# One queue for the first loads, two score tiles ahead of the block means: a fused attention, mixture-of-experts and feed-forward kernel

## The reference, cut to what matters

```python
# q, k, v: [2, 8, 768, 64]; block 32, window 16
k_sum = k.reshape(B, H, nb, 32, D).max(axis=3)       # 24 block maxima of the keys
v_sum = v.reshape(B, H, nb, 32, D).mean(axis=3)      # 24 block means of the values
scores_l = where(|i - j| < 16, scale * q @ k.T, -1e9)
scores_s = scale * q @ k_sum.T + log(32)
a = softmax(concat([scores_l, scores_s]))            # +1e-9 in the denominator
x = a @ concat([v, v_sum])                           # -> [1536, 512]
logits = x @ w_gate; noisy = logits + log1p(exp(x @ w_noise)) * noise
top 2 of 8 experts per token, softmax of the two noisy logits
x = sum over the two: weight * (relu(x @ w1[e]) @ w2[e])     # 512 -> 1024 -> 512
out = (s * relu(x @ w_in)**2 + b) @ w_out                    # 512 -> 2048 -> 512
```

## Time and profile before

| | us |
|---|---|
| median of 3 runs | 733.51 |
| the profiled execution, whole | 733.46 |
| its span in the trace | 731.8 |
| PE busy in the span | 692.8 (95%) |
| DVE, ACT, POOL busy | 263.7, 215.0, 294.2 |
| mean granted TensorE clock | 0.978 of full |

### The profile page before, as it was taken

How to read it: one execution, slowest core, us unless ns; L and a number is a source line. 1 busy time by engine, 2 the same in 40 slices (tenths; PEclk the granted TensorE clock), 3 DMA queues, 4 the chain that set the end, 5 groups by cost and what they waited for, 6 DMA issues and landing times.

```text
span 731.8 us, 10317 instructions
## 1 busy us (share of the span) xinstructions
PE 692.8 (95%) x4019; PEld 566.6 (77%) x4022; DVE 263.7 (36%) x535; ACT 215.0 (29%) x503; POOL 294.2 (40%) x273
## 2 busy tenths in 40 slices
PE   8888867999999999999999998999999999999993
PEld 3466653878888888887989897888888888888883
DVE  3557777581111211211111235845505235152220
ACT  0678961112031221212121212412315123242120
POOL 0001554478978667394979750502031020200002
PEclk9999977999999999999999999999999999999997
DMA  9994986963969679393989695942011020100001
GB/s 234 238 249 118 305 299 222 366 239 118 330 209 356 210 255 357 117 394 129 331 273 365 196 384 224 374 154 58 0 61 56 0 58 1 57 1 1 0 1 57
DMA packets 57291, 135.35 MB, mean 185 GB/s; under 512 B 9437, under 2 KB 11741, under 8 KB 57245
## 3 DMA queue, kind: packets, MB, share of 16 engines
q0 software_dynamic: 30288, 88.13, 35.4%
q1 hardware_dynamic: 25760, 44.24, 19.7%
q10 hardware_dynamic: 1197, 2.36, 1.3%
HBM read 108.99 MB, written 24.67 MB: 183 GB/s over the span
## 4 chain that ended last, share of the span: by engine, by line
PE 79%; DMA 7%; DVE 4%; SPq 4%; ACT 2%; issue 2%; POOL 1%; POOLq 0%; DVEq 0%
PE ps L335 24%; PE ps L336 24%; PE ps L337 24%; DMA v_all<-in_v_dram 3%; DMA yg<-y_sorted,ord_i 2%; PE ps L1313 2%; SPq L316 1%; PE ps L1261 1%; PE ps L1244 1%; POOL x_sorted L480 1%; SPq L350 1%; SPq L311 1%; ACT prob L597 1%; DMA y_sorted<-ysb 1%; PE ps L1399 1%
## 5 line engine op out<-in xcount | busy, mean ns | idle before, releaser
L460 POOL TENSOR_TENSOR w_lo<-w_raw,w_hi 128x1024 fp32r<-128x1024 f32 x56 | 133.5, 2425 | 27.8 <-DVE w_lo L812 15.1
L1038 DVE SCALAR_TENSOR_TENSOR h_lo<-ps,h_hi 128x448 fp32r<-128x448 f32 (+1 forms) x64 | 38.1, 598 | 206.6 <-ACT h_hi L647 206.6
L335 PE MATMUL ps<-w_hi,h_hi 128*128 128x512 f32 x232 | 93.2, 402 | 0.0
L335 PE MATMUL ps<-x_hi,w_hi 128*128 128x448 f32 (+1 forms) x256 | 91.6, 358 | 1.3 <-DVE x_lo L1032 1.3
L647 ACT ACTIVATE h_hi<-ps 128x448 fp32r<-128x448 f32 (+1 forms) x64 | 33.6, 525 | 196.3 <-PE ps L337 196.3
L336 PE MATMUL ps<-x_lo,w_hi 128*128 128x448 f32 (+1 forms) x256 | 91.1, 356 | 0.0
L337 PE MATMUL ps<-x_hi,w_lo 128*128 128x448 f32 (+1 forms) x256 | 91.0, 356 | 0.0
L336 PE MATMUL ps<-w_lo,h_hi 128*128 128x512 f32 x232 | 90.8, 392 | 0.0
L337 PE MATMUL ps<-w_hi,h_lo 128*128 128x512 f32 x232 | 90.8, 391 | 0.0
L1117 DVE SCALAR_TENSOR_TENSOR sqr<-relu,sbb 128x512 f32<-128x512 f32 x48 | 36.2, 754 | 113.0 <-ACT relu L700 112.2
L336 PE MATMUL ps<-y_lo,w_hi 128*128 128x512 f32 (+1 forms) x200 | 76.1, 381 | 0.0
(11 more groups left out here) (197 smaller groups left out, 1088.5 us busy)
## 6 DMA issues: line engine op xcount, KB each, us to landing
w_hi<-in_w_pieces_dram POOLq DMA_DIRECT2D x64, 512.0 KB, 14.1
w_raw<-in_w_pieces_dram POOLq DMA_DIRECT2D x56, 512.0 KB, 13.5
x_sorted<-zrow SPq DMA_DIRECT2D x8, 896.0 KB, 15.3
xb<-x_sorted SPq DMA_DIRECT2D x24, 256.0 KB, 8.0
y_sorted<-ysb SPq DMA_DIRECT2D x24, 256.0 KB, 2.0
w_raw<-in_w_pieces_dram SPq DMA_DIRECT2D x8, 512.0 KB, 5.8
w_hi<-in_w_in_dram POOLq DMA_DIRECT2D x8, 512.0 KB, 10.1
w_raw<-in_w_in_dram SPq DMA_DIRECT2D x8, 512.0 KB, 15.7
```

Of the source, the lines that this page charges most:

```text
L335: pe.matmul(acc, l_hi, r_hi, start=start, stop=False, skip_group_check=True)
L460: pool.tensor_tensor(piece(w_lo, slot, k), piece(w_raw, slot, k), piece(w_hi, slot, k).bitcast(F32), ALU.subtract).then_inc(pieces_split, 1)
L1038: dve.scalar_tensor_tensor(out=h_lo[:, at, i % FT, 0:rows], in0=ps[:, i % FT, 0:rows], scalar=0.0, in1=h_hi[:, at, i % FT, 0:rows].bitcast ...
```

## The change

SP now issues all first loads; ACT issues none. The values of batch 0 stand behind `ident`, first as 80 rows of each window (what the means need) and then the remaining 16 as a DMA of its own (`halo_in`). The values of batch 1 come ahead of its keys, and `noi` and `sbb` behind the first halves of its queries, with a semaphore `n_in` of their own that DVE waits for in `route_top`. On PE, `scores(0)`, `scores(1)` and `turn_probs(0)` come ahead of `means(0)`; the warm-up is 34, 8 and 6 matmuls in three places where it was 66 in one; the means of batch 0 go to PSUM banks 6 and 7, and sum over 80 rows. DVE, not ACT, copies the means of batch 0. The key maxima of batch 1 move from tiles 1, 2, 3, 4 to 2, 3, 3, 4. ACT's first act is a small copy, after the zeros of `zrow` are there.

```diff
--- before.py
+++ after.py
...
+MEAN_ROWS = HALF + 16
+MEAN_BANKS = ((6, 7), (2, 1))
+KEY_SUMS_AT = (2, 3, 3, 4)
...
+        n_in, halo_in = sem("n_in"), sem("halo_in")
...
@@ -298,10 +302,13 @@
         def overflow_steps(eng):
             return eng.value_load(t_last[0:1, 0:1], min_val=0, max_val=OVER)
 
-        def load_values(eng, b):
-            windows = bass.AP(tensor=v.tensor, offset=v[b].offset, ap=[[DM, HALF + 32], [HALF * DM, HPB - 1], [1, DM]])
+        def load_windows(eng, b, at, to, landed):
+            windows = bass.AP(tensor=v.tensor, offset=v[b, at].offset, ap=[[DM, to - at], [HALF * DM, HPB - 1], [1, DM]])
+            eng.dma_start(v_all[b][at:to, 0:HPB - 1, :], windows).then_inc(landed, 16)
+
+        def load_values(eng, b, rows):
             last = (HPB - 1) * HALF
-            eng.dma_start(v_all[b][0:HALF + 32, 0:HPB - 1, :], windows).then_inc(v_in[b], 16)
+            load_windows(eng, b, 0, rows, v_in[b])
             eng.dma_start(v_all[b][0:HALF, HPB - 1, :], v[b, last:last + HALF, :]).then_inc(v_in[b], 16)
             eng.wait_ge(init_ready, 1)
             eng.dma_start(v_all[b][HALF:WKEYS, HPB - 1, :], v[b, S:S + 2 * PAD, :]).then_inc(v_in[b], 16)
@@ -344,13 +351,15 @@
             sp.dma_start(msk[0:80, :], masks[0:80, :]).then_inc(m_in, 16)
             load_queries(sp, 0, 0)
             sp.dma_start(ident[:, :], consts[:, 0:P]).then_inc(id_in, 16)
+            load_values(sp, 0, MEAN_ROWS)
+            load_windows(sp, 0, MEAN_ROWS, HALF + 32, halo_in)
             load_queries(sp, 0, 1)
             sp.dma_start(wg[:, :, :], w_gate.rearrange("(k p) e -> p k e", p=P)).then_inc(g_in, 16)
-            sp.dma_start(noi[:, :, :], noise.rearrange("(t p) e -> p t e", p=P)).then_inc(g_in, 16)
-            sp.dma_start(sbb[:, :], s_b).then_inc(g_in, 16)
+            load_values(sp, 1, HALF + 32)
             load_keys(sp, 1)
-            load_values(sp, 1)
             load_queries(sp, 1, 0)
+            sp.dma_start(noi[:, :, :], noise.rearrange("(t p) e -> p t e", p=P)).then_inc(n_in, 16)
+            sp.dma_start(sbb[:, :], s_b).then_inc(n_in, 16)
             load_queries(sp, 1, 1)
             sp.wait_ge(init_ready, 2)
             clear_rows(sp, 0)
@@ -585,9 +594,8 @@
 
             def copy_means(b):
                 act.wait_ge(means_done, b + 1)
-                if b == 1:
-                    act.wait_ge(rows_done, 1)
-                act.activation(vs_sb[:, :], ps[:, 2, :], ACT.Copy).then_inc(vs_ready, 1)
+                act.wait_ge(rows_done, b)
+                act.activation(vs_sb[:, :], ps[:, MEAN_BANKS[b][0], :], ACT.Copy).then_inc(vs_ready, 1)
 
             def exps(s):
                 act.wait_ge(nb_ready, s + 1)
@@ -607,10 +615,10 @@
                 act.wait_ge(ln_in, g + 1)
                 act.activation(rt[:, R_LN, 0:to - at, :], rt[:, R_Y, 0:to - at, :], ACT.Ln).then_inc(ln_ready, 1)
 
-            load_values(act, 0)
+            act.wait_ge(init_ready, 2)
+            act.activation(gate[:, :], zrow[:, 0:NT], ACT.Copy)
             key_windows(0)
             key_windows(1)
-            copy_means(0)
             exps(0)
             ends = {to: g for g, (at, to) in enumerate(GROUP_OF)}
             for s in range(NT + 1):
@@ -802,9 +810,13 @@
                 dve.tensor_copy(sel[:, 0:NSUM].rearrange("p (c m) -> p c m", m=NSUM // KD),
                                 ident[:, :].rearrange("p (c m) -> p c m", c=KD)[:, :, 0:NSUM // KD]).then_inc(sel_ready, 1)
 
+            def copy_means(b):
+                dve.wait_ge(means_done, b + 1)
+                dve.tensor_copy(vs_sb[:, :], ps[:, MEAN_BANKS[b][0], :]).then_inc(vs_ready, 1)
+
             def mean_rows(b):
                 dve.wait_ge(rows_done, b + 1)
-                dve.tensor_copy(v_all[b][SUMS:COLS, 0:2 - b, :], bc(ps[SUMS:COLS, 3 - 2 * b, :], 2 - b, 1)).then_inc(rows_ready, 1)
+                dve.tensor_copy(v_all[b][SUMS:COLS, 0:2 - b, :], bc(ps[SUMS:COLS, MEAN_BANKS[b][1], :], 2 - b, 1)).then_inc(rows_ready, 1)
 
             def split_first(k):
                 dve.wait_ge(raw_first[k], 16)
@@ -859,6 +871,7 @@
                 n = to - at
                 dve.wait_ge(lg_ready, to)
                 dve.wait_ge(ln_ready, g + 1)
+                dve.wait_ge(n_in, 32)
                 link(dve.tensor_tensor(rt[:, R_SP, 0:n, :], rt[:, R_LN, 0:n, :], rt[:, R_C, 0:n, :], ALU.subtract))
                 link(dve.tensor_tensor(rt[:, R_N, 0:n, :], rt[:, R_SP, 0:n, :], noi[:, at:to, :], ALU.mult))
                 link(dve.tensor_tensor(rt[:, R_L, 0:n, :], rt[:, R_N, 0:n, :], lg[:, at:to, 0:E], ALU.add))
@@ -900,9 +913,8 @@
             key_sums(1)
             masks_to_bf16()
             select_rows()
+            maxima(0)
             token_numbers()
-            maxima(0)
-            mean_rows(0)
             for s in range(NT):
                 if s in (7, 10):
                     route_chosen(s // 10)
@@ -910,8 +922,12 @@
                     maxima(s + 1)
                 dve.wait_ge(turned, 2 * s + 1)
                 dve.tensor_copy(probT[0:COLS, 0:4, :], ps[0:COLS, 4, :].rearrange("p (h n) -> p h n", n=P)).then_inc(probT_even, 1)
-                if 1 <= s <= PAIRS:
-                    summary(1, s - 1)
+                if s == 0:
+                    copy_means(0)
+                    mean_rows(0)
+                for p in range(PAIRS):
+                    if s == KEY_SUMS_AT[p]:
+                        summary(1, p)
                 if s in (TPB - 2, TPB - 1):
                     key_sums(s + 2)
                 if s == 4:
@@ -1177,8 +1193,6 @@
                 pe.wait_ge(sums_ready, 2 * b + min(tt, 1) + 1)
                 if s >= 2:
                     pe.wait_ge(exps_done, 8 * (s - 1))
-                if s == 1:
-                    pe.wait_ge(rows_ready, 1)
                 if s == TPB - 1:
                     pe.wait_ge(vs_ready, 2)
                 if s == TPB:
@@ -1202,7 +1216,8 @@
                 pe.wait_ge(v_in[b], 48)
                 for r in range(HPT):
                     for c in range(KD):
-                        mm = pe.matmul(ps[c * 32:c * 32 + 32, 2, :], amean[0:WKEYS, r, :], v_all[b][0:WKEYS, c * HPT + r, :],
+                        mm = pe.matmul(ps[c * 32:c * 32 + 32, MEAN_BANKS[b][0], :], amean[0:MEAN_ROWS, r, :],
+                                       v_all[b][0:MEAN_ROWS, c * HPT + r, :],
                                        start=(r == 0), stop=(r == HPT - 1), skip_group_check=True)
                 mm.then_inc(means_done, 1)
 
@@ -1210,7 +1225,7 @@
                 if b == 0:
                     pe.wait_ge(sel_ready, 1)
                 pe.wait_ge(vs_ready, b + 1)
-                pe.matmul(ps[SUMS:P, 3 - 2 * b, :], sel[:, :], vs_sb[:, :], start=True, stop=True).then_inc(rows_done, 1)
+                pe.matmul(ps[SUMS:P, MEAN_BANKS[b][1], :], sel[:, :], vs_sb[:, :], start=True, stop=True).then_inc(rows_done, 1)
             def warm_up(count, bank):
 
                 pe.wait_ge(init_ready, 1)
@@ -1230,6 +1245,8 @@
                 b, tt = divmod(s, TPB)
                 if tt == 0:
                     pe.wait_ge(rows_ready, b + 1)
+                if s == 0:
+                    pe.wait_ge(halo_in, 16)
                 if tt == 1 - b:
                     pe.wait_ge(means_in[b][0], 16)
                 if tt == 3:
@@ -1255,7 +1272,7 @@
 
             def logits(t):
                 if t == 0:
-                    pe.wait_ge(g_in, 48)
+                    pe.wait_ge(g_in, 16)
                 pe.wait_ge(xT_ready, t + 1)
                 for k in range(KD):
                     mm = pe.matmul(ps[:, 7, 0:2 * E], xT[:, t % 2, k, :], wg[:, k, :], start=(k == 0), stop=(k == KD - 1))
@@ -1273,17 +1290,21 @@
                     mm = pe.matmul(acc, ones[:, :], before[:, t, :], start=False, stop=True)
                 mm.then_inc(rank_done, 1)
 
-            warm_up(66, 7)
+            warm_up(34, 7)
+            scores(0)
+            scores(1)
+            warm_up(8, 7)
+            turn_probs(0)
+            warm_up(6, 7)
             means(0)
-            scores(0)
             gather_means(0)
-            for s in range(NT):
+            values(0)
+            for s in range(1, NT):
                 if s + 1 < NT:
                     scores(s + 1)
-                if s >= 1:
-                    if s in (8, 11):
-                        pe.wait_ge(rank_read, 1 + s // 11)
-                    turn_x(s - 1)
+                if s in (8, 11):
+                    pe.wait_ge(rank_read, 1 + s // 11)
+                turn_x(s - 1)
                 turn_probs(s)
                 if s == 3:
                     means(1)
@@ -1292,8 +1313,7 @@
                 if s in (7, 10):
                     pe.wait_ge(xT_ready, s)
                     ranks(s // 10)
-                if s >= 1:
-                    logits(s - 1)
+                logits(s - 1)
                 values(s)
             turn_x(NT - 1)
             logits(NT - 1)
```

## The result

The changed kernel takes 743.4 us (median of 6 runs) against 733.15 in the same group: 1.0121 of before, 95% interval 1.0083 to 1.0159. Forecast were 729.3 us, between 726.2 and 732.8. The ratio leaves out one run of 798.05 us, taken in a slower state of the chip (granted clock 0.829). The profiled execution has a span of 742.2 us where it was 731.8, and a mean granted clock of 0.955 where it was 0.978.

A forecast was written before the change was run, and what follows sets the result against it. Attention tiles were taken as bound by PE's own order, with time to win only at the start and where PE waits: 2.3 - 0.2 + 2.13 = 4.2 us off 733.46 gives 729.3 us, range 726.2 to 732.8.

The forecast's parts named there:

- That is reached at 20.4 + 0.11/0.354: Start: the 4.90 MB up to the batch-0 values are in at 20.7 us if nothing overtakes.
- I take 21.7: Landing of the batch-0 values, chosen between 20.7 us without overtaking data and 22.6 with the same overhang as before.
- The 6.2 us from means to values: Batch-0 chain of means, DVE copy, gather and DVE write: 6.2 us, so values of tile 0 start at 28.2.
- I take the middle, 6.6: Spread of the 192 KB of mean rows ahead of tile 1's values: 6.6 us, between bounds 4.3 and 8.9.
- The estimate of at most 6.9 us: Spread beside packets of its own size at most doubled, 6.9 us; the sum would then be 0.3 us less.
- the wait for the spread covers that price: Ahead of tile 1's values: a fallen clock makes PE ready at 34.9 instead of 33.2, hidden as the spread ends later.
- Rival B: Spread keeps 8.9 us, no gain at the start, 2.1 in tile 3, half clock may return for a tile: 731.3 us, chance 0.17.
- The 0.2 us for late keys: Tile 2: DVE waits 0.9 us for batch-1 keys against 0.65 of slack, losing 0.2 us of the start's gain.
- The 2.13 us go whole: Tile 3: PE's 2.13 us wait for the batch-1 values ahead of their means disappears entirely.
- I let a shift of tile 4 pass to the end whole: Beyond tile 4: later work is released by counts of finished tiles, so the shift reaches the end undiminished.
- which bytes come first, not how many pass in a us: Start: with DMA engines full, putting loads on one queue changes only their order, not the rate.
- rival C: Slower: batch-0 values land late behind 2.8 MB on one queue; at 190 GB/s they land at 27.8, 735.3 us, chance 0.09.

The follow-up runs named there:

- e5: Kernel before with only the batch-0 values moved from ACT's queue to SP's, behind the identity, 96 rows in one DMA: 764.0 us, 1.0128.
- e6: Changed kernel with the batch-0 values on ACT's queue, issued once the second key piece is in: 763.91 us, 1.0133.
- e14: Changed kernel, unchanged, measured again on another chip: 764.13 us, 1.0125 of the kernel before.
- e3: Changed kernel with PE's idle time in the start filled by matmuls of zeros: 738.25 us, 1.0061 of the kernel before.
- e2: Changed kernel with the two small batch-0 value pieces issued ahead of the large one: 741.4 us, 1.0084 of the kernel before.
- e1: Kernel before with only the batch-1 half of the change (values ahead of keys, noise and scale behind queries, later key maxima): 734.38 us, 1.0015.
- e8: Changed kernel with the large DMA of batch-0 values cut into 11, one a window: 760.13 us, 1.0103 of the kernel before.
- e4: Changed kernel with ACT copying the means' rows into windows 2 and 3, the DMA spread only from window 4 on: 736.16 us, 1.0006.
- e9: Changed kernel with rows of windows 2 and 3 by ACT and PE's idle time filled with matmuls of zeros: 755.51 us, 1.0050.
- e12: Kernel before with DVE copying rows into windows 2 and 3, idle PE time filled, and the batch-1 half of the change: 752.36 us, 0.9995.
- e15: Changed kernel with window 2 and 3 rows by ACT, idle filled, values loaded window by window, key maxima in tiles 3, 3, 4, 4: 749.26 us, 0.9942.
- e16: Kernel before with window 2 and 3 rows by DVE, idle filled and the batch-1 half, repeated on another chip: 750.04 us, 0.9956.
- The four runs on one chip: Kernel before, changed kernel, and the two repaired kernels e15 and e16, unchanged, on one chip: ratios 0.9953, 1.0125, 0.9942, 0.9956.
- e13: Kernel before, unchanged, measured again against itself on another chip: 753.43 us, 0.9953.

## Why the prediction was wrong

The order of things was read rightly: the wait ahead of the first scores (2.5 us forecast, 2.62 measured), the wait of tile 1 for the spread, and the stall ahead of the means of batch 1, which went. Three of the signs of being wrong came too: means later than 24 us, tile 1 later than 36.5, and stretches beyond tile 4 longer by over 1 us. The values of tile 1 were put at 35.05 us; they came at 44.38, and the 9.3 us come from these steps:

- **Landing of the batch-0 values, 3.4 us.** "That is reached at 20.4 + 0.11/0.354": the rate behind 20.4 us was taken from a stretch of queries. With values moving it was 167 GB/s. The 212 GB/s of the values' own stretch stood in the earlier trace rows, and the prediction used it for batch 1 and not here. The other half of the miss is "I take 21.7", the middle between no overhang and 0.67 MB. With 212 in its formula the middle is 22.5 and the full overhang 24.1 us; with 167 and the full overhang it is 25.1. The landing was at 25.3, behind 0.8 MB of later data, so the overhang came whole. Against the 22.0 that PE's order allowed the means came 3.4 us later. PE itself was ready only at 23.05, as its clock was at half from 16 to 20 us, behind the first wait; that is within the price given ("23.6 at most") and hidden by the landing. e5 shows the place in the order as the cause, e6 that a second queue is no remedy.
- **Clock on the chain, 2.2 us.** The 6.2 us from means to values were counted at full clock; they took 8.4, and 8.9 in e14. A fallen clock was priced for the scores and never for the means and the gather, which stand behind a wait too. With the idle time filled they took 6.05 us (25.00 to 31.05, e3). The size is that of an execution: in e2, unfilled, they took 6.02 and the fall came just behind them.
- **Spread, 3.7 us.** "I take the middle, 6.6": it took 10.3, above the upper bound of 8.9, and 10.0 to 11.3 in every run that spread 192 KB beside values (e1 to e3, e5 to e8, e14). The reason given, shorter packets beside it, was no measurement. Nor does the time go with the size, as the prediction's scaling by 192/240 assumed: cut to 96 KB the copy took 8.1 to 10.2 us (e4, e9 to e12, e15, e16). The Trainium skill (DMA: Bandwidth & Descriptors, "Queues, rings and completion order") has each DMA engine take turns between its queues, a packet from each. The estimate of at most 6.9 us was worked out from that rule and took the packets of both queues as equal, which no run shows; the measurement decides, and by it that estimate is too low here.

Then, "the wait for the spread covers that price" had it the other way round: the clock had come back at 40 us, fell again at 43.5 in the wait for the spread, and tile 1 took 2.6 us more for it. Rival B said that half the clock may return for a tile there, and gave it no price. The 0.2 us for late keys did not come, as tile 2 was late itself; e9 shows that wait, 3.07 us, once the rest is repaired. "The 2.13 us go whole" held, 2.25 us with the tile's length. So tile 4 is 7.46 us late where 4.2 were to be won: 9.3 + 2.6 - 0.2, 11.7 us apart.

Last, "I let a shift of tile 4 pass to the end whole" is wrong by 3 us, and the granted clock was lower in both stretches beyond tile 4; no run isolates that as the cause. The four runs on one chip show that such a shift can grow or shrink.

One sentence behind the sum is wrong as well: "which bytes come first, not how many pass in a us". From 2 to 8 us the changed kernel moved 314 GB/s and the one before 217, at shares of 0.98 and 1.01, and e5, which differs from the kernel before in the place of the values alone, moved 307. By 20.4 us the two were even again. Two slips change nothing: the scores with the whole overhang come out at 15.9 us, not 15.5, and the 235 GB/s of rival C counts from 0 us where its 190 counts from 2, where it would be 260.

Rival C was the nearest, with 0.09: the values late behind 2.8 MB. Its mechanism is right (e5), but it put the turn at a landing of 26 us. With a spread of 10.3 us, 6.05 us from means to values and the 2.25 us won in tile 3, an estimate of the turn is a landing near 23 us at full clock (37.33 + 2.25 - 10.3 - 0.3 - 6.05 - 0.1 = 22.8), and earlier with the fallen clock. The rivals were priced one by one, while late values, idle PE, fallen clock and an exposed DMA follow from one another. No run has PE's new order with the values issued first by ACT, so what that order is worth by itself is not shown.

## What to carry to other kernels

Before a transfer is moved to a shorter path, ask what hid it: here one tile's work less ahead of it exposed an SBUF-to-SBUF DMA that takes 10 us beside full queues and could be replaced by a 1 us copy on ACT (1.05 us in e4). Price a wait of TensorE twice, once for itself and once for the half clock that may follow on whatever comes behind it: here waits of 1.7 to 2.7 us had it behind them in some executions and not in others. Take the rate of a transfer from a stretch in which that very data moves, and count the whole overhang of later data. And before a shift of 1 us is read from one execution, look how far unchanged code moves between two.

## What was not expected of the hardware

- With all 16 DMA engines at a share of 1.05 to 1.1, the rate was 354 GB/s for mostly queries, 212 for batch-1 values and 135 to 184 for the end of the batch-0 values (after, e3, e4, e9, e14). Why is open; cutting the load by windows gave 246, 225 and 239 GB/s from 14 to 20 us in place of 211 to 216, with no sooner landing in two of the three.
- A 192 KB copy within SBUF landed after 8.9 and 8.5 us beside keys (before, e13) and 10.0 to 11.3 beside values, one of 96 KB after 8.1 to 10.2. One of 240 KB beside an empty queue took 4.3 to 5.5.
- One program, the kernel before, had its clock fall at 27.9 us in one execution, behind a wait of 1.66 us, and kept it full behind a wait of 2.13 ahead of 48.58. In another (e13) it kept it full behind the same 1.66 us and fell at 48, behind 2.41. The two were 1.6 us apart at tile 0.
